# Two matrix products by seven block products: the block sums chained and shared, weights staged in two homes

## The reference

```python
def _attn_ref(q, k, v, tau):
    scale = 1.0 / np.sqrt(q.shape[-1])
    scores = scale * np.matmul(q, k.transpose(0, 1, 3, 2))
    thresh = np.max(scores, axis=-1, keepdims=True) - tau
    scores = np.where(scores >= thresh, scores, -1000000000.0)
    ...
    return np.matmul(attn, v).astype(np.float32)
...
x = attn_out.transpose(0, 2, 1, 3).reshape(B * S, H * D)
h = x @ moe_w_in;  x = (h - np.tanh(h)) @ moe_w_out
h = x @ moe2_w_in; x = (h * (1.0 / (1.0 + np.exp(-h)))) @ moe2_w_out
```

## Time and profile before

| | before |
|---|---|
| median of 3 runs | 1135.16 us (1131.64 to 1136.63) |
| profiled execution, its own time | 1134.14 us |
| span of its trace | 1132.3 us |
| busy: PE, DVE, ACT, POOL | 91%, 77%, 61%, 43% |
| mean granted TensorE clock | 0.964 of full speed |
| chain of work that ended last, its PE part | 37% of the span |

### The profile page before, as it was taken

The page is one execution under the profiler, slowest core; times in us unless marked ns, Lnnn a source line. Parts: engine busy times, 40 slices in busy tenths (PEclk is TensorE's granted clock), DMA queues, the critical chain, the costliest instruction groups (busy, mean ns, idle before and its releaser), DMA issues. The chain is left out here.

```text
span 1132.3 us, 18009 instructions
## 1 busy us (share of the span) xinstructions
PE 1033.3 (91%) x6004; PEld 932.4 (82%) x6004; DVE 874.7 (77%) x1678; ACT 688.2 (61%) x1346; POOL 489.0 (43%) x522
## 2 busy tenths in 40 slices
PE   4899999999887889986799888999999999999998
PEld 3667676666576879976799788999999998999898
DVE  6899998899756789566897778965699458955486
ACT  5899998998745455345463555636655465536443
POOL 6999998996844420245300453004500352005100
PEclk9999999999988899998999899999999999999999
DMA  7145345423216457254484542834267434834076
GB/s 269 57 178 191 138 168 184 148 71 117 65 47 230 159 185 257 86 214 143 139 267 159 192 142 94 266 125 149 76 215 230 154 106 136 260 127 168 19 249 216
DMA packets 57883, 181.00 MB, mean 160 GB/s; under 512 B 5056, under 2 KB 6592, under 8 KB 57792
## 3 DMA queue, kind: packets, MB, share of 16 engines
q1 hardware_dynamic: 57504, 179.78, 46.7%
q10 hardware_dynamic: 288, 0.07, 0.0%
HBM read 145.75 MB, written 34.08 MB: 159 GB/s over the span
## 5 line engine op out<-in xcount | busy, mean ns | idle before, releaser
L1314 PE MATMUL b<-x_op,w_op 128*128 128x384 f32 x2016 | 380.2, 350 | 45.2 <-DVE b L1073 32.9
L1314 PEld LDWEIGHTS b<-x_op,w_op 128*128 128x128 f32 x2016 | 371.0, 199 | 52.8 <-DVE b L1073 36.5
L1390 PE MATMUL b<-g_op,w 128*128 128x384 f32 x2016 | 362.0, 340 | 23.1 <-DVE g_op L1121 14.8
L1390 PEld LDWEIGHTS b<-g_op,w 128*128 128x128 f32 x2016 | 355.6, 191 | 29.2 <-issue 18.9
L588 POOL TENSOR_TENSOR w_sum<-w_raw 128x256 f32<-128x256 f32 x48 | 37.0, 771 | 395.9 <-PE b L1314 395.9
L847 ACT ACTIVATE g_op<-g_sum 128x768 fp32r<-128x768 f32 x120 | 101.7, 848 | 139.4 <-DVE g_sum L1107 129.3
L967 DVE TENSOR_SCALAR_CACHE_REDUCE probs<-scores,fine 128x576 f32<-128x576 f32 x144 | 116.9, 812 | 15.7 <-PE scores L1275 15.3
L1275 PEld LDWEIGHTS scores<-k_lo,q_parts 128*128 128x128 f32 x336 | 64.7, 195 | 71.2 <-issue 40.1
L1275 PE MATMUL scores<-k_lo,q_parts 128*128 128x288 f32 x336 | 107.4, 343 | 17.3 <-DVE q_parts L1011 7.3
L999 DVE SCALAR_TENSOR_TENSOR probs<-scores,stats,probs 128x576 f32<-128x576 f32 x144 | 117.8, 818 | 0.1
L620 POOL TENSOR_SCALAR probs<-probs,rinv 128x576 f32<-128x576 f32 x144 | 108.8, 756 | 20.0 <-DVE rinv L992 13.3
(11 more groups left out here) (84 smaller groups left out, 1345.7 us busy)
## 6 DMA issues: line engine op xcount, KB each, us to landing
w<-scr SPq DMA_DIRECT2D x168, 512.0 KB, 4.4
w_raw<-w_in SPq DMA_DIRECT2D x56, 512.0 KB, 3.4
scr<-w_op SPq DMA_DIRECT2D x8, 1792.0 KB, 8.4
scr<-stage SPq DMA_DIRECT2D x8, 1792.0 KB, 7.0
k_raw<-k_in SPq DMA_DIRECT2D x15, 576.0 KB, 5.7
q_raw<-q_in SPq DMA_DIRECT2D x15, 576.0 KB, 7.0
v_all<-v_in SPq DMA_DIRECT2D x16, 320.0 KB, 3.1
stage_raw<-w_in SPq DMA_DIRECT2D x8, 512.0 KB, 7.9
```

The lines of the kernel that those rows point to most:

```text
L1314: last = pe.matmul(out, a, b, start=fresh and k == 0 and i == 0, stop=k == 1 and i == 2, skip_group_check=True)
L1390: last = pe.matmul(bank[n][kind], x, y, start=fresh and q == 0 and f == 0 and i == 0, stop=q == 3 and f == 1 and i == 2, skip_group_check= ...
```

## The change

**The scheme.** The seven products are now those of Winograd's form. Four block sums are made instead of five, each from the one before: for weights S = w22 + w21 kept as slot 3, then S - w11, w12 - that, w11 - w22. Three operands are raw blocks. The same goes for x (`X_SUMS`, where `None` names an earlier sum) and for g, where the sums of products 5 and 6 are written over the tile c12 in place. In PSUM m1 is copied by ACT to a second bank (`seed`), m6 and m7 are accumulated there, ACT keeps copies of m5 (`take_s5`) and of m1 + m6 (`take_u2`), and DVE adds them (`add_u2`, `add_s5`). The copies have two buffers each. The number of matmuls of 384 columns stays 4032.

**The staging.** The second layer's weights go two blocks a pass in four passes, through two buffer pairs; the second pair lies over the projection's weight buffers, so their loads wait for its store. SP loads both blocks at the start of a pass. In attention the pieces begin at step 12 instead of 2, there are 8 for each of 9 blocks: the ninth is the weights of job 0, which before were made after step 144. SP stores a block at a pair start and no longer up to four steps behind it. A job's weights are made one job ahead, not two. The x operands of pass 0 are spread over the tail of attention (`TAIL_HI`), and DVE's preparation of tau comes after its first three splits.

```diff
 def free_steps(late):
 
-    return [n for n in range(2, STEPS * BATCH) if split_in(n % STEPS - late, n < STEPS)[0] is None]
-
-
-PIECES = 9
+    return [n for n in range(12, STEPS * BATCH) if split_in(n % STEPS - late, n < STEPS)[0] is None]
+
+
+PIECES = 8
+STAGED = FP + 1
 POOL_STEPS = free_steps(1)
 ACT_STEPS = free_steps(0)
 
 
...
-    if n not in POOL_STEPS or POOL_STEPS.index(n) >= PIECES * FP:
+    if n not in POOL_STEPS or POOL_STEPS.index(n) >= PIECES * STAGED:
...
-STAGE_AT = [next(g for g in range(2, PAIRS * BATCH) if TILES * g + 4 >= POOL_STEPS[PIECES * f + PIECES - 1] or g == PAIRS * BATCH - 1)
+X_SUMMED = (5, 6, 4, 7)
+X_SUMS = {5: (0, 1, 0, 0, ALU.subtract), 6: (1, 1, None, 5, ALU.subtract), 4: (1, 0, None, 6, ALU.subtract),
+          7: (1, 1, 0, 1, ALU.subtract)}
+G_SUMS = {5: ("12", "11"), 6: ("22", "12"), 7: ("12", "11"), 4: ("21", "12")}
+NEXT = (0, 1), (2, 3), (4, 5), (6, 7)
+NEXT_HOME = {f: i % 2 for fs in NEXT for i, f in enumerate(fs)}
+NEXT_BEFORE = {f: max(e for e in range(f) if NEXT_HOME[e] == NEXT_HOME[f]) for f in range(FP) if f not in (0, 1)}
+NEXT_COUNT = {f: sum(NEXT_HOME[e] == NEXT_HOME[f] for e in range(f + 1)) for f in range(FP)}
+STAGE_AT = [next(g for g in range(2, PAIRS * BATCH) if TILES * g >= POOL_STEPS[PIECES * f + PIECES - 1] or g == PAIRS * BATCH - 1)
             for f in range(FP)]
-TAIL_SUMS = {STEPS: (4,), STEPS + 2: (3,), STEPS + 4: (1,), STEPS + 6: (6,), STEPS + 8: (7,)}
-X_SUM_AT = {2: (4,), 3: (3,), 6: (1,), 9: (6,), 11: (7,)}
-X_HI_AT = {6: (5, 4), 9: (2, 3), 12: (1,), 14: (6,), 15: (7,)}
-X_LO_AT = {13: (5, 4), 14: (2, 3), 15: (1,), 16: (6,), 26: (7,)}
+TAIL_SUMS = {STEPS: (5,), STEPS + 2: (6,), STEPS + 4: (4,), STEPS + 6: (7,)}
+TAIL_HI = (1, 1), (5, 4), (6, 6), (2, 9), (3, 10), (7, 12), (4, 14)
+X_SUM_AT = {1: (5,), 2: (6,), 9: (4,), 13: (7,)}
+X_HI_AT = {3: (1, 5), 7: (6,), 10: (2,), 11: (3,), 14: (7,), 15: (4,)}
...
+                    load_next(z, f)
                 for j in range(FP):
-                    if j % 2 == 0 and j // 2 < len(nexts):
-                        load_next(z, nexts[j // 2])
-                    if j == 1:
+                    u = FP * z + j + 2
+                    if u < JOBS:
+                        load_w(u)
+                    if j >= 2 and j % 2 == 0 and j // 2 <= len(nexts):
+                        store_next(nexts[j // 2 - 1])
+                    if j == FP - 3:
                         for i in range(W2_SLOTS):
                             load_w2(BATCHES * z + i)
-                    if j < FP - 1 and FP * z + j + 4 < JOBS:
-                        load_w(FP * z + j + 4)
-                    if j % 2 == 1 and j // 2 < len(nexts):
-                        store_next(nexts[j // 2])
                 for i in range(W2_SLOTS, BATCHES):
...
+            def sums_of(raw, sums, done, base):
+
+                def total(slot, a, b, how):
+                    pool.tensor_tensor(sums[:, slot, 1], a, b, how).then_inc(done, 1)
+
+                total(3, raw[:, 3], raw[:, 2], ALU.add)
+                pool.wait_ge(done, base + 1)
+                total(4, sums[:, 3, 1], raw[:, 0], ALU.subtract)
+                pool.wait_ge(done, base + 2)
+                total(5, raw[:, 1], sums[:, 4, 1], ALU.subtract)
+                total(6, raw[:, 0], raw[:, 3], ALU.subtract)
...
-                                   x_block(0, k1, t1), how).then_inc(x_sums, 1)
-
...
+            def w_sums_of(u):
+                pool.wait_ge(w_loaded[u % 2], 16 * ((u + 1) // 2))
+                if u == 1:
+                    pool.wait_ge(stage_stored[1], 8 * FP)
+                else:
                     pool.wait_ge(m7_done, u - 1)
-                pool.tensor_tensor(sums[:, 5, 1], raw[:, 2], raw[:, 0], ALU.subtract).then_inc(w_sums, 1)
-                pool.tensor_tensor(sums[:, 6, 1], raw[:, 1], raw[:, 3], ALU.subtract).then_inc(w_sums, 1)
+                sums_of(w_raw[u % 2], w_sum[u % 2], w_sums, 4 * (u - 1))
 
             def next_sums_of(f):
-                pool.wait_ge(next_loaded, 16 * (f + 1))
-                if f > 0:
-                    pool.wait_ge(next_stored, 16 * f)
...
-            def take_t5(u):
+            def seed(u):
+                z, j = divmod(u, FP)
+                act.wait_ge(m1_done, u + 1)
+                if j >= 2:
+                    act.wait_ge(c_done, 4 * (u - 2) + C_POS["21"] + 1)
+                elif z > 0:
+                    act.wait_ge(y_by_act, 4 * (z - 1) + 3 + j)
+                act.activation(bank[u % 2]["21"], bank[u % 2]["11"], ACT.Copy).then_inc(seed_done, 1)
+
+            def take_s5(u):
                 act.wait_ge(m5_done, u + 1)
-                if u > 0:
-                    act.wait_ge(seed11_done, u)
-                if u % FP == 0 and u > 0:
-                    act.wait_ge(p_seed11_done, 2 * (u // FP))
-                act.activation(t5[:], bank[u % 2]["12"], ACT.Copy).then_inc(t5_taken, 1)
-
...
+            def take_u2(u):
+                act.wait_ge(m6_done, u + 1)
+                if u >= 2:
+                    act.wait_ge(c12_done, u - 1)
+                act.activation(u2[u % 2][:], bank[u % 2]["21"], ACT.Copy).then_inc(u2_taken, 1)
...
                 if z < SPLITS:
                     if n >= 2:
...
                     act.wait_ge(c_done, 4 * (FP * z + 2 * q + 1) + C_POS[kind] + 1)
                     if z < len(NEXT) and gb % BATCHES in range(1, G_SLOTS):
-                        act.wait_ge(next_stored, 16 * (NEXT[z][-1] + 1))
+                        f = max(f for f in NEXT[z] if NEXT_HOME[f] == 0)
+                        act.wait_ge(next_stored[0], 16 * NEXT_COUNT[f])
                     source = c_tile(kind, z, 2 * q, 2)
                 act.activation(g_op[gb % G_SLOTS][:, 0], source, ACT.Copy).then_inc(g_hi, 1)
 
             def hidden(z):
-                take_t5(FP * z)
                 for j in range(FP):
                     u = FP * z + j
-                    if 2 <= u + 1 < JOBS:
-                        w_hi_b(u + 1)
-                    if u + 2 < JOBS:
-                        w_hi_raw(u + 2)
-                    if j + 1 < FP:
-                        take_t5(u + 1)
-                    if j == 0:
-                        take_c21(u)
-                        nonlinear("21", u)
-                        nonlinear("12", u)
-                    if u + 2 < JOBS:
...
+            def add_u2(u):
+                dve.wait_ge(u2_taken, u + 1)
+                dve.wait_ge(m3_done, u + 1)
+                tile = bank[u % 2]["12"]
+                dve.tensor_tensor(tile, tile, u2[u % 2][:], ALU.add).then_inc(c12_done, 1)
+
+            def add_s5(u):
                 z, j = divmod(u, FP)
-                dve.wait_ge(t5_taken, u + 1)
-                dve.wait_ge(m4_done, u + 1)
-                if j >= 2:
-                    dve.wait_ge(c_done, 4 * (u - 2) + C_POS["11"] + 1)
-                elif z > 0:
-                    dve.wait_ge(y_by_act, 6 * (z - 1) + 5 + j)
-                dve.tensor_tensor(bank[j % 2]["11"], bank[j % 2]["21"], t5[:], ALU.subtract).then_inc(seed11_done, 1)
-
...
                     return
...
+            def need_w(u, part):
+                if u == 0:
+                    pe.wait_ge(stage_lo, 4 * STAGED)
+                else:
+                    pe.wait_ge(w_split, 4 * (u - 1) + part)
+
+            def m1_m5(u):
                 z, j = divmod(u, FP)
-                pe.wait_ge(w_split, 3 * u + 2)
+                need_w(u, 1)
                 if j >= 2:
-                    pe.wait_ge(c_done, 4 * (u - 2) + C_POS["12"] + 1)
-                    pe.wait_ge(diff_done, u - 1)
+                    pe.wait_ge(c_done, 4 * (u - 2) + C_POS["11"] + 1)
                 elif z > 0:
-                    pe.wait_ge(y_by_act, 6 * (z - 1) + 1 + j)
+                    pe.wait_ge(y_by_act, 4 * (z - 1) + 1 + j)
                 elif j == 0:
                     pe.wait_ge(lift_done, SCORED)
                     pe.wait_ge(x_split, 1)
-                    touch(0, "11")
-                    touch(0, "22")
...
-                    pe.wait_ge(c_done, 4 * (u - 2) + C_POS["21"] + 1)
-                    pe.wait_ge(c21_taken, u - 1)
-                elif z > 0:
-                    pe.wait_ge(y_by_act, 6 * (z - 1) + 3 + j)
-                product_of(4, u, bank[j % 2]["21"], True, m4_done)
-
-            def m2_m3(u):
-                pe.wait_ge(seed11_done, u + 1)
-                product_of(2, u, bank[u % 2]["21"], False, m2_done)
+                need_w(u, 4)
+                pe.wait_ge(c22_done, u + 1)
+                product_of(4, u, bank[u % 2]["21"], False, m4_done)
+
+            def m6_m2_m3_m7(u):
+                pe.wait_ge(seed_done, u + 1)
+                product_of(6, u, bank[u % 2]["21"], False, m6_done)
+                product_of(2, u, bank[u % 2]["11"], False, m2_done)
+                pe.wait_ge(s5_taken, u + 1)
+                need_w(u, 3)
                 product_of(3, u, bank[u % 2]["12"], False, m3_done)
-
...
```

(11 more changed lines are left out.)

623 lines of the change are left out of this document (293 added, 330 removed).

## The result

The changed kernel takes 1049.16 us (median of 4 runs, 1045.60 to 1049.38) against 1135.25 for the kernel before on the same chip: ratio 0.924, interval 0.921 to 0.927. The forecast was 1044 with the range 1022 to 1080, and faster with 0.97. The profiled execution took 1049.05 us, its span is 1047.2, 85 us under the profiled execution of before.

What follows compares the result with a forecast made beforehand. PE bounds the layers, losing 102 of 809 us to waits of order and latency; attention's body has four full engines. 1134.1 less 74 (layers) less 16 (attention) gives 1044 us, range 1022 to 1080.

Steps and rivals of the forecast that it cites:

- The step of 7.3 us: Hidden part: seven products of 1.05 us each on PE, with ACT's copies covered and u2's copy having 0.8 us slack.
- m4 behind the staged low parts: Passes with staging: m4 waits 1.3 us behind the first block's low parts, 1.9 behind the second's.
- the slow rival: Hidden steps: POOL's four chained sums, stretched by the port shared with DVE, stall every step; 1141 us, chance 0.02.
- the other two late loads: Job loads behind SP's stores, besides the next pass's first: they fall into time m4's waits already lost, costing nothing.
- The 0.9 at m7 of job 7: Step of job 7: the next pass's first load, behind store and projection loads, makes ACT's copy 0.9 us late.
- 1.6 us a drop: Passes 0 to 2: one drop to the lower PE clock after a wait in each, costing 1.6 us.
- 6.5 and 3, less 1: Attention: 6.5 from early DVE and PE waits gone, 3 from earlier stores, 1 lost to more POOL units.
- the 7 at the end: End of attention: PE's 4.92 us wait for an ACT copy goes, plus part of 2.05 and weight copies; 7 us.
- ACT as bound: Rival: in all hidden steps ACT's PSUM copies wait for PE, needing 8.1 us a step; 1073 us, chance 0.16.
- A loose timetable: Rival: waits of about 1 us are covered and no clock drop comes, passes 0 to 3 119 to 120; 1025, chance 0.20.
- Attention did give: Denies a rival: attention's body, paced by four full engines, takes back what the gaps give; 1060 us, chance 0.09.
- the second staged block does not wait for its load: Denies a rival: that block waits 6.17 us for its load in each of four passes; 1068 us, chance 0.05.

Runs made afterwards that it cites:

- x2: The changed kernel without staging the second layer's weights in the passes (the layer computes with the first layer's); 1010.43 us, ratio 0.890.
- x7: The changed kernel with SP's staged stores one step later, behind the job load, and projection loads at step 6, behind the next pass's first load; 1028.27 us.
- x4: The changed kernel with attention's staged pieces from step 2 and the stores four steps later, as before; 1062.22 us, ratio 0.935.
- x12: The changed kernel with ACT's seven x copies at the end of attention late again (tail steps 8 to 14); 1048.47 us, ratio 0.926.
- x8: x7 with DVE's three low-part instructions of a staged block split over two steps; 1028.96 us, ratio 0.909.
- x5: The changed kernel with POOL's sums of the second staged block in step 1 of a pass instead of step 2; 1043.96 us.
- x6: The changed kernel with DVE's low parts of a staged block ahead of the job's own instead of behind them; 1023.65 us, ratio 0.904.
- x10: The changed kernel with both edits of x5 and x6; 1018.70 us, ratio 0.898.

## Why the prediction was right, and where not

- **Sum.** 90 us foreseen, 85 came: the layers 69.3 by the windows (74 foreseen), attention the other 15.9 (16 foreseen). By PE's own first matmul of the layers, 319.29 us in the kernel before, attention gave 15.1. Small slips of the working do not move the forecast: the first three passes hold 84 us of waits, not 85, and 117.8 + 0.4 + 0.5 is 118.7, not 118.8.
- **Scheme of seven products.** The step of 7.3 us with every copy covered is right: x2 has 1.6 us of idle time in the 48 steps. The projection's 0.5 for x's sums did not come; the pass start's 0.4 is one wait of 0.82 in passes 4 and 5 and none before; passes 4 and 5 were foreseen at 118.8 and take 117.5 and 117.8.
- **m4 behind the staged low parts.** Mis-sized. The prediction took 2.4 us for a staged block's low parts and 0.70 for 512 columns of the job's, and 1.3 us of wait. Both are right where POOL is idle (2.24 and 0.68 to 0.69 in x7); beside POOL the seven together take 8.06 us instead of 4.7, and the wait is 2.9 to 3.5. It had named the port, but let it count only in the slow rival, at every step. The stretch does show at other steps (1.22 instead of 0.68 at 439.51 and 483.90), but makes m4 wait only where a staged block's low parts follow. That passes 0 and 2 came out near the forecast (124.6 and 124.4 against 125.4 and 124.9) is in part luck: the first wait was too small by 1.6 to 2.2 us, the second, foreseen at 1.9, did not come.
- **SP.** The prediction saw that each store precedes a job's load and said that "the other two late loads fall into the time that m4's waits have lost anyway: nothing". That step failed: x7 takes these loads, and the next pass's first, out of the stores' way, and 21 us go. The late load shifts POOL's sums onto DVE's low parts, which takes time from both, and the next m4 and m7 are late. The 0.9 at m7 of job 7 was 1.1 to 2.4. That a load behind a store does not overtake it is borne out: 9.5 us from the issue to POOL's start, against 3.4 for a load alone.
- **Pass 3** was foreseen at 122.3 since DVE has no gates there. It took 127.6. In place of gates DVE waits for ACT's first high part of the job, which stands behind the copy of m5 whether DVE has gates or not: 2.50 us in step 2, where the staged block's copies stand ahead of it on ACT, and as long (2.49) in step 1, where none do, so the staged block is not the reason. Then the low parts, slowed as in pass 1 (1.30 instead of 0.69), end as late as there, 25.3 us into the pass:

```profile
690.61 0.71 DVE L1027 TENSOR_TENSOR w_op<-w_raw,w_op 128x512 fp32r<-128x512 f32 x1 [2.49 <-ACT w_op L779]
...
698.20 1.30 DVE L1027 TENSOR_TENSOR w_op<-w_raw,w_op 128x512 fp32r<-128x512 f32 x1 [2.50 <-ACT w_op L779]
...
697.54 0.63 ACT L779 ACTIVATE w_op<-w_raw 128x512 fp32r<-128x512 f32 x1
```

- **Clock.** 1.6 us a drop for three passes, 4.8 in all, was foreseen. The price was right, the count was not: there are four drops, one in each of passes 0 to 3, the fourth in pass 3, for which none was in the sum. Two of them (windows, PE alone: us, busy, PEclk, DMA share, GB/s):

```profile
456.00:461.00 5.00, 5.00 (x22) 0.66 1.01 325
...
746.00:751.00 5.00, 4.42 (x16) 0.66 0.00 0
```

  5 us at a mean of 0.66 are 1.7 us lost; the four together cost 6.4 us of matmul time.
- **Attention.** Right in sum, and in part by luck. Until the layers begin PE idles 27.3 us before (319.29 less 292.01 busy) and 15.5 after (304.20 less 288.72); the other 3.3 of the 15.1 us are shorter matmul time, and the prediction had no term for the clock here. Before, it has a mean of 0.57 in 30:34, 0.66 in 200:205 and 0.53 in 313:320; after, it falls once (0.66 in 295:300). x4 says that the pieces' place gives 11.6; the prediction had 8.5 for it (6.5 and 3, less 1). So at most 4 us are left for tau and the end, where 7.5 were foreseen: that is the term that was too large. The wait of 4.92 did not go whole, three gaps of 2.27 us in all stand there, and the four early x copies, part of the 7 at the end, give nothing (x12). Tau's place was not tried alone; the first scores start at 6.00 us instead of 7.27, so it may hold 1.3 (foreseen 1).
- **Rivals.** ACT as bound, 1073, needed waits for its copies in every step: passes 4 and 5 have one of 0.82 each. A loose timetable, 1025: the scheme is that loose, the staging isn't. Attention did give, POOL's chain does not stall at every step, and the second staged block does not wait for its load (POOL makes its sums at 445.78, right behind those of job 3). The split of the staging into two homes works as said: without it 27 us are back.

## What to carry to other kernels

A store in an in-order queue that waits for late work holds back every load behind it, and the wait that it makes appears two engines further on, under another name: before pricing a late load at nothing, follow it to the next step's operand. Put filler work (here the low parts of a staged block) ahead of the engine's own, where it can fall into a wait that exists anyway, if what comes behind still has slack; and do not let two engines that slow each other do their filler in the same step. A kernel without the filler work shows what is left to win: here 39 us, of which reordering alone won 35.

## What had not been expected of the hardware

The same gaps are followed by a lower clock in one run and not in another. At the end of attention the changed kernel and x7 have the same code and the same gaps of 0.60 and 1.11 us; the window there (PE alone; us, busy, PEclk, DMA share, GB/s) is, in the changed kernel and in x7:

```profile
293.00:299.00 6.00, 4.29 (x23) 0.78 0.01 3
```

```profile
293.00:299.00 6.00, 4.53 (x33) 1.00 0.01 3
```

One profile drops to a mean of 0.78 in these 6 us and begins its first pass at 304.20, the other stays at 1.00 and begins at 302.34. x8, with the same work up to there, drops too (0.77) and begins at 304.11; x5, x6 and x10 begin at 302.42 to 302.68. So 1.7 us of a difference between two single profiles of these kernels may be this alone. The largest gap ahead of the drop was 1.11 us. Why the same gaps are followed by a drop in some profiles and not in others was not settled.
